# A two-layer network behind channel attention: the first layer from seven block products instead of eight

## What is computed

```python
# q, k, v: (2, 6016, 256); w_in: (256, 2048); w_out: (2048, 256); alpha: (2048,)
qn = q / (norm of q over the 6016 tokens + 1e-6);  kn the same for k
s = kn.transpose(0, 2, 1) @ qn / tau          # 256 x 256 for each batch
a = softmax(s, last axis)
x = (v @ a).reshape(12032, 256)
h = x @ w_in
g = np.maximum(h, 0) + alpha * np.minimum(h, 0)
y = g @ w_out                                  # (12032, 256)
```

## Time and profile before

| | |
|---|---|
| median of three runs | 1151.94 us (1149.97 to 1152.36) |
| span of the profiled execution, first to last instruction | 1147.4 us |
| PE busy | 1134.5 us, 99% of the span |
| DVE busy | 840.3 us, 73% |
| ACT busy | 551.0 us, 48% |
| DMA | 54.6 MB, 13.0% of 16 engines |

### The profile page before, as it was taken

The page is one execution under the profiler, slowest core; times in us unless marked ns, Lnnn a source line. Parts: engine busy times, 40 slices in busy tenths (PEclk is TensorE's granted clock), DMA queues, the critical chain, the costliest instruction groups (busy, mean ns, idle before and its releaser), DMA issues.

```text
span 1147.4 us, 15404 instructions
## 1 busy us (share of the span) xinstructions
PE 1134.5 (99%) x5218; PEld 952.6 (83%) x5220; DVE 840.3 (73%) x1297; ACT 551.0 (48%) x944; POOL 1.3 (0%) x8
## 2 busy tenths in 40 slices
PE   8999999999999999999999999999999999999998
PEld 6778888888888888888898888888888888888888
DVE  5788768678687696876867777767667667667666
ACT  5664545536455454454544544444444444444443
POOL 0000000000000000000000000000000000000000
PEclk9999999999999999999999999999999999999999
DMA  8720210202102012012011010110110110110100
GB/s 307 297 92 1 74 67 9 73 0 73 73 0 73 27 46 73 0 73 73 0 37 33 1 37 1 37 37 0 37 37 0 37 37 0 37 37 0 37 19 15
DMA packets 15308, 54.63 MB, mean 48 GB/s; under 512 B 1584, under 2 KB 2096, under 8 KB 12336
## 3 DMA queue, kind: packets, MB, share of 16 engines
q1 hardware_dynamic: 15280, 54.28, 13.0%
HBM read 41.95 MB, written 12.32 MB: 47 GB/s over the span
## 4 chain that ended last, share of the span: by engine, by line
PE 93%; DVE 3%; DMA 2%; ACT 1%; issue 1%; SPq 0%; ACTq 0%; DVEq 0%
PE y_ps L444 43%; PE h_ps L423 43%; PE s_ps L345 3%; DMA stage<-qk 2%; PE s_ps L323 2%; PE h_ps L392 1%; DVE g L761 1%; DVE g_lo L647 1%; PE small_ps L392 0%; DVE g_hi L771 0%; DVE acc L683 0%; ACT sq L547 0%; DVE sq L713 0%; ACT h_pos L584 0%; DVE col L717 0%
## 5 line engine op out<-in xcount | busy, mean ns | idle before, releaser
L761 DVE SCALAR_TENSOR_TENSOR g<-h_neg,neg_alpha,h_pos 128x512 f32<-128x512 f32 (+1 forms) x384 | 284.1, 740 | 222.6 <-ACT h_neg L585 205.5
L584 ACT ACTIVATE h_pos<-h_ps 128x512 f32<-128x512 f32 (+1 forms) x384 | 226.6, 590 | 453.8 <-PE h_ps L423 282.5
L444 PE MATMUL y_ps<-g_hi,w_hi 128*128 128x512 f32 (+1 forms) x768 | 296.5, 386 | 1.3 <-DVE g_lo L647 1.3
L444 PE MATMUL y_ps<-g_hi,w_lo 128*128 128x512 f32 (+1 forms) x768 | 295.8, 385 | 0.0
L444 PE MATMUL y_ps<-g_lo,w_hi 128*128 128x512 f32 (+1 forms) x768 | 295.3, 384 | 0.0
L647 DVE TENSOR_TENSOR g_lo<-g,g_hi 128x512 fp32r<-128x512 f32 (+1 forms) x384 | 261.8, 682 | 13.3
L585 ACT ACTIVATE h_neg<-h_ps 128x512 f32<-128x512 f32 (+1 forms) x384 | 224.6, 585 | 0.0
L771 DVE CAST g_hi<-g 128x512 fp32r<-128x512 f32 (+1 forms) x384 | 161.9, 422 | 34.6
L444 PEld LDWEIGHTS y_ps<-g_hi,w_hi 128*128 128x128 f32 x768 | 144.3, 188 | 28.4 <-DVE g_lo L647 2.2
L444 PEld LDWEIGHTS y_ps<-g_lo,w_hi 128*128 128x128 f32 x768 | 144.2, 188 | 27.7
L444 PEld LDWEIGHTS y_ps<-g_hi,w_lo 128*128 128x128 f32 x768 | 144.4, 188 | 25.8
(11 more groups left out here) (85 smaller groups left out, 647.9 us busy)
## 6 DMA issues: line engine op xcount, KB each, us to landing
stage<-qk SPq DMA_DIRECT2D x23, 1024.0 KB, 6.3
v_stage<-v_tiles SPq DMA_DIRECT2D x24, 512.0 KB, 3.8
y_t<-y_stage SPq DMA_DIRECT2D x22, 512.0 KB, 3.0
y_stage<-w_pieces SPq DMA_DIRECT2D x8, 512.0 KB, 5.8
stage<-qk SPq DMA_DIRECT2D x2, 512.0 KB, 4.5
y_t<-y_stage SPq DMA_DIRECT2D x2, 384.0 KB, 2.5
tau_sb<-tau_col SPq DMA_DIRECT2D x1, 0.5 KB, 5.0
alpha_sb<-alpha_cols SPq DMA_DIRECT2D x1, 8.0 KB, 5.2
```

Source lines behind the costliest of these rows:

```text
L444: product = nc.tensor.matmul(y_ps[oc][:, 0:width], w_part[:, piece, ws], g_part[:, j % GBUF, 0:width], start=(j == 0 and w_part is w_hi an ...
L584: nc.scalar.activation(h_pos[:, 0:width], h, ACT.Relu)
L761: nc.vector.scalar_tensor_tensor(out=g[:, 0:width], in0=h_neg[:, 0:width], scalar=neg_alpha[:, j:j + 1], in1=h_pos[:, 0:width], op0=ALU.mu ...
```

## The change

The kernel is rewritten around a different unit of work. A tile is now two halves of 512 tokens (1024 tokens; 6 tiles for each batch, the last one with halves of 448). A **group** is one tile and one pair of feature blocks (`jp`, 8 per tile, 96 groups in all). The up product of a group is a 2 x 2 by 2 x 2 block product: features × channels by channels × tokens. It is done by Strassen's method (Winograd's form) with 7 block products of three matmuls each, and no longer with 8:

- `mix_m` forms four sums of M's blocks (S1 to S4) and `mix_v` four sums of v's blocks (T1 to T4) on DVE. ACT and DVE split all seven operands on each side.
- Four products are added up, one after the other, in one PSUM bank X. ACT copies the running sum out after each (`take_x`, L572), since each is a part of one of the four results. Bank Y gets one product, bank Z two, one on top of the other; DVE adds them to what ACT took (`add_part`, L767).
- The slope becomes max(h, alpha·h) on DVE (`slope`, L775), one instruction from SBUF. Where alpha is above 1, signs are turned by a factor `sigma`, which is also put on w_out.
- The layer's second product (`down`, L406) runs one group behind, in four parts that stand between the seven up products.
- M is made by exact fp32 matmuls, 8 steps of 4 (`make_m`, L378); for batch 2 one step stands in each of the groups 41 to 48. The q·k products of batch 2 are exact too: 11 blocks in the head (`late_blocks`), 18 pairs of blocks at the end of groups 8 to 25. The norms and the softmax of batch 2 stand in groups 32 to 37.
- All loops are unrolled. The loads come in other pieces: q and k of batch 1 in 13, v as two per tile, w_in whole (2 MB) before the first `make_m`, w_out in four parts.

The diff of what the prediction speaks of:

```diff
-                    for j in range(FJ):
-                        up(j)
...
-                        if j >= LAG:
-                            down(j - LAG)
+            for G in range(GROUPS):
+                T, jp = G // JP, G % JP
+                if jp == 0:
+                    pe.wait_ge(v_lo_ready, NOP * (T + 1))
+                if T % TILES == 0:
+                    pe.wait_ge(m_lo_ready, JP * (T // TILES) + jp + 1)
+                if G > 0:
+                    pe.wait_ge(c11_done, G)
...
+                up(T, jp, Y, A12, B21, True).then_inc(y_done, 1)
...
+                    pe.wait_ge(x_copied, 4 * G)
+                up(T, jp, X, A11, B11, True).then_inc(x_done, 1)
+                if G > 0:
+                    pe.wait_ge(c12_done, G)
+                up(T, jp, Z, S1, T1, True).then_inc(z_done, 1)
+                if G > 0:
+                    down(G - 1, 0)
+                pe.wait_ge(x_copied, 4 * G + 1)
+                up(T, jp, X, S2, T2, False).then_inc(x_done, 1)
+                if G in M_AT:
+                    pe.wait_ge(c11_done, G + 1)
+                    pe.wait_ge(slice_loaded[M_AT[G] % 2], 16 * (M_AT[G] // 2 + 1))
+                    make_m(Y, w_slice[:, M_AT[G] % 2, :, :])
...
+                if G > 0:
+                    down(G - 1, 1)
+                pe.wait_ge(x_copied, 4 * G + 2)
+                up(T, jp, X, S3, T3, False).then_inc(x_done, 1)
+                if G > 0:
+                    down(G - 1, 2)
+                pe.wait_ge(x_copied, 4 * G + 3)
+                up(T, jp, X, A22, T4, False).then_inc(x_done, 1)
+                pe.wait_ge(c22_done, G + 1)
+                up(T, jp, Z, S4, B22, False).then_inc(z_done, 1)
+                if G > 0:
+                    down(G - 1, 3)
```

```diff
+            def take_x(G, n, k):                       # ACT
...
+                act.wait_ge(x_done, 4 * G + n + 1)
+                if G > 0:
+                    act.wait_ge(g_lo_ready, 4 * (G - 1) + k + 1)
...
+                nc.scalar.mul(h[:, k, 0:H], X[:, 0:H], sigma[:, j:j + 1]).then_inc(x_copied, 1)
...
+                take_x(G, 0, 0)
+                if G > 0:
+                    split_g_hi(G - 1, 3)
+                if jp == 1 and T > 0:
+                    take_y(T - 1, 1)
+                take_x(G, 1, 3)
...
+                if G in M_AT:
+                    take_m(1, M_AT[G])
+                take_x(G, 2, 1)
+                split_g_hi(G, 0)
+                take_x(G, 3, 2)
+                split_g_hi(G, 1)
+                split_g_hi(G, 2)
+                if jp == 0 and T > 0:
+                    take_y(T - 1, 0)
+                if G in M_AT:
+                    split_m_hi(1, M_AT[G])
+                if G in W_OUT_AT:
+                    split_w_hi(W_OUT_AT[G])
```

```diff
+        W_OUT_AT = {2 * n - 1: n for n in range(1, FJ // 4)}
+        V_DVE = {1: (B11, "T1"), 2: (B22, "T3"), 3: (T1, "T2"), 4: (T3,), 5: (T2, B21, "T4"), 7: (T4,)}
...
+            mix_m(0, 0)                                # DVE, batch 1
+            for jp in range(JP):
+                if jp + 1 < JP:
+                    mix_m(0, jp + 1)
+                split_m_lo(0, jp)
+            dve.wait_ge(sigma_ready, 1)
+            split_w_lo(0)
```

More of the change, by code:

```diff
@@ L164, in blocks @@
[L164 to L176, removed]
-        def tiles(eng, b, body):
-            body(0, 0, 0, True, False)
-            with eng.Fori(0, PAIRS) as i:
-                body(i * 2 + 1, i, 1, False, False)
-                body(i * 2 + 2, i + 1, 0, False, False)
-            body(TILES - 1, TILES // 2 - 1, 1, False, True)
@@ L186, in groups @@
[L186 to L196 removed]
+        v_mixed = sem("v_mixed")
+        v_hi_ready = sem("v_hi_ready")
+        v_lo_ready = sem("v_lo_ready")
+        x_done = sem("x_done")
+        y_done = sem("y_done")
@@ L297, in _ @@
+            store(ALL - 1, 0)
+            store(ALL - 1, 1)
+            for t in range(2):
+                sp.wait_ge(y_stored[t], 16 * ALL)
         @block.gpsimd
@@ L351, in channel_sums, with late_blocks @@
-            def channel_sums(b):
-                pe.wait_ge(folded, b + 1)
+                        s_ps[b][:, kc * C:(kc + 1) * C], rows[:, C + kc * P:C + (kc + 1) * P], rows[:, 0:C],
+                        start=False, stop=last, skip_group_check=True)
+                return product
+            def late_blocks(n0, n1):
+                for n in range(n0, n1):
+                    for part in range(len(LATE_PARTS)):
+                        if n == sum(LATE_PARTS[:part]):
+                            pe.wait_ge(late_loaded[part], 16)
+                    product = qk_block(1, late[:, n, :], False)
+                    if n == LATE - 1:
+                        product.then_inc(qk1_summed, 1)
@@ L354, in channel_sums @@
+            def channel_sums(b):
+                acc = (acc0, acc1)[b]
+                if b == 0:
+                    pe.wait_ge(acc0_done, len(SUBS))
+                else:
+                    pe.wait_ge(acc1_done, len(LATE_SUBS) + PAIRS)
                 for n in range(2 * CC):
-                    sums = nc.tensor.matmul(sums_ps[:, n:n + 1],
-                                            acc[:, n // CC, 0, (n % CC) * P:(n % CC + 1) * P],
-                                            ones[:, 0:1], start=True, stop=True)
+                    for half in range(2):
+                        sums = nc.tensor.matmul(sums_ps[:, n:n + 1], acc[:, half, n * P:(n + 1) * P],
+                                                ones[:, 0:1], start=half == 0, stop=half == 1)
@@ L490, in _, with make_m @@
-            product.then_inc(qk_summed, 1)
-            for b in range(B):
-                make_m(b)
-                tiles(pe, b, body(b))
+                moved.then_inc(at_moved, 1)
+            def make_m(bank, w_of):
+                for kc in range(CC):
+                    for qc in range(CC):
+                        product = nc.tensor.matmul(
+                            bank[:, kc * 2 * P:(kc + 1) * 2 * P], at[:, qc, kc * P:(kc + 1) * P], w_of[:, qc, :],
+                            start=qc == 0, stop=qc == CC - 1, skip_group_check=True)
+                product.then_inc(m_done, 1)
@@ L496, in _ @@
+            for k in range(4):
+                down(GROUPS - 1, k)
         @block.scalar
         def _(act):
-            def square(n, t, b, slot, nblk, anew):
-                if not anew:
-                    act.wait_ge(acc_done, t * 2 + (2 * TILES * b + n - 1))
-                nc.scalar.activation(sq[:, n, 0:nblk, :], stage[:, slot, n, 0:nblk, :],
-                                     ACT.Square).then_inc(sq_ready, 1)
-            def split_v(T, par):
-                act.wait_ge(v_loaded, T * 16 + 16)
-                nc.scalar.copy(v_hi[:, par, :, :], v_stage[:, :, :]).then_inc(v_hi_ready, 1)
@@ L636, in _ @@
+            split_g_hi(GROUPS - 1, 3)
+            for t in range(2):
+                take_y(ALL - 1, t)
         @block.vector
```

999 lines of the change are left out of this document (524 added, 475 removed).

## The result

The change takes **1210.22 us** (median of 4 runs, 1207.3 to 1213.03), against 1152.03 us before, measured beside it: ratio 1.051, 95% interval 1.049 to 1.0531. It is slower, as forecast, but 22 us above the forecast's 1188 and 8 us above the likeliest case's own range (1172 to 1202). It lies in the range of 1160 to 1212 by 2 us, and two of the four runs (1212.7 and 1213.03) do not. By its number it is nearest to the rival of the missing spare (1205, 0.12), which the trace excludes, and 8 us from the rival *the clock falls at every pause* (1218, 0.05), to which the trace points.

A forecast was written before the change was run, and what follows sets the result against it. PE's count of matmuls was taken as the bound. 88.3 us to X2, 1008.0 of remaining PE work and waits (13.7, 29.6, 33, 3.5, 1.2, 1.4, 4.4) gave a 1183.1 span; 4.5 more made 1188, range 1160 to 1212.

The forecast's parts named there:

- the likeliest case: Whole kernel: the forecast as walked, 1188 us with 1172 to 1202 as its own range, chance 0.66.
- the rival of the missing spare: Plain groups: the 0.3 us spare before Z2 is absent, some 85 groups stall 0.2 each, +17, 1205 us; chance 0.12.
- the clock falls at every pause: PE's pauses of 2.9 us and more, some 19 places: half speed costs 1.6 each, +30, 1218 us; chance 0.05.
- A plain group: A group without extra work: runs in 10.20 us without a stall, tightest spare 0.3 us before Z2.
- DVE drains faster: DVE's slopes, additions and splits: follow each other at 0.43 us, not 0.60 to 0.66; 38 less, 1150 us; chance 0.14.
- Tile starts: Eleven tile starts: Y waits for v's last split, 2.9 us each, 3.3 behind a q·k pair, sum 29.6.
- Batch 2's M: Groups 41 to 49: the chain of sums, cast and split delays the fourth `g_lo` and `make_m`, sum 33 us.
- Batch 1's M: Head: two buffers, 3.2 us a part; X2 starts at 88.3, PE idles 12.1 us.
- Tile 0: First tile: uncovered copies, slow clock, squares, additions and w_out pieces delay its groups, sum 13.7 us.
- I add 8 x 0.2 = 1.6: Tile 0, after the pause behind batch 1's M: first matmuls at the 1.2 GHz level cost 1.6 us.
- The 4.5 us from span to median: Whole kernel: the runs' median stands 4.5 us above the span, taking 1183.1 to 1188.
- It does not save matmuls: Whole kernel: rival that matmuls are not saved; excluded, since PE's order has 45 in a group.

The follow-up runs named there:

- experiment 6: The changed kernel with zero matmuls in the pause behind batch 1's M, at each tile start and in groups 41 to 48: 1194.13 us.
- experiment 5: The changed kernel with zero matmuls in PE's waits in the groups around batch 2's M, 8 ahead of X2 and 5 ahead of `make_m`: 1203.52 us.
- experiment 3: The changed kernel with 45 zero matmuls in the pause behind batch 1's M: 1204.7 us.
- experiment 2: The changed kernel with ten zero matmuls ahead of PE's wait at each tile start: 1204.69 us.
- The fastest version: The changed kernel with splits, squares and sums moved into waits, more buffers for both batches' M, and 20 zero matmuls behind batch 1's M: 1116.15 us.
- experiment 4: The changed kernel with two buffers for batch 2's M, its sums and splits one group after `make_m`: 1175.38 us.

## Why the prediction was right and where not

The sum can be held against the trace stretch by stretch, from one start of a Y product in the timeline to another (us; the first column is put together from the terms of the sum and, rounded, adds up to 1183.9; the last is experiment 6):

| stretch | walked | the change | experiment 6 |
|---|---|---|---|
| start to tile 1 | 179.0 | 181.7 | 182.3 |
| tile 1 | 100.2 | 100.9 | 99.4 |
| tile 2 | 100.2 | 101.1 | 99.4 |
| tile 3 | 88.5 | 91.0 | 88.2 |
| tile 4 | 89.4 | 91.6 | 90.1 |
| groups 40 to 49 | 140.5 | 156.1 | 145.9 |
| groups 50 to 55 | 64.1 | 64.2 | 64.2 |
| tiles 7 to 10 | 340.0 | 341.2 | 341.1 |
| tile 11 to the end | 82.0 | 83.7 | 84.1 |

- **A plain group, 10.20.** Measured 10.20. The rival *the spare is not there* falls: in plain groups neither X3 nor Z2 waits. Pair groups 11.94 (11.97 walked).
- **Slope and additions.** They have the duration of the instruction taken for them. By line and form, x count | busy us, mean ns:

```profile
L775 DVE SCALAR_TENSOR_TENSOR h<-h,alpha_sb 128x512 f32<-128x512 f32 x320 | 232.2, 747 | 2.8
L767 DVE SCALAR_TENSOR_TENSOR h<-z_ps,sigma,h 128x512 f32<-128x512 f32 x160 | 120.1, 751 | 146.8 <-ACT h L572 145.9 <-PE z_ps L386 0.9
L767 DVE SCALAR_TENSOR_TENSOR h<-p_ps,sigma,h 128x512 f32<-128x512 f32 x80 | 59.6, 746 | 0.0
L760 DVE TENSOR_TENSOR m_lo<-mf,m_hi 128x896 fp32r<-128x896 f32 x16 | 17.4, 1089 | 8.0 <-ACT m_hi L560 8.0
```

  So the rival *DVE drains faster* falls. Reading PSUM costs no more than SBUF here: 751 and 746 against 747 ns. The surcharge that the Trainium skill gives (VectorE: DVE Perf Modes, TRN2 errata) isn't seen in this instruction. The 896-wide split was walked at 1.09 and takes 1.089.
- **Tile starts, 2.9 each.** 2.7 to 2.8 (12.97 - 10.20) eight times, 3.36 (15.3 - 11.94) for the two behind a q·k pair, 3.3 walked, all released by `v_lo` as said. The eleventh is group 48's.
- **Batch 2's M.** The walk gives 93.8 us for the groups 42 to 47 with the wait at group 48's start (6 x 10.79 of matmuls + 23.1 + 6.0). At full clock they take 94.6, in experiments 5 and 6 both. The fourth `g_lo` of group 42 ends 6.98 us into the next group (620.23 of 613.25, experiment 5's group 43), walked 5.8 + 2 x 0.54 = 6.88. ACT's copy ahead of X2, for which the walk had nothing, costs next to nothing at full clock, since `make_m` right behind it waits longer. So the stall was sized rightly; in the change, with the clock's fall, the same groups take 105.7.
- **Batch 1's M.** X2 at 89.09 for 88.3, parts 3.12 us apart for 3.2.
- **Tile 0.** Walked stalls 3.4, 3.2, 1.0 and 2.3 in groups 1, 2, 4 and 6; measured 3.4, 3.9, 1.0 and 2.4.
- **What failed** is the step "I add 8 x 0.2 = 1.6", and with it the 0.05 for the clock at every pause. I put the clock's fall into the sum once, where it was known that PE had stood still for 12 us, and took a wait of 1.81 us with full speed behind it as evidence for all the others. The tile starts' were longer, 2.54 us and up, and at the starts of tiles 1 to 5 half speed stood behind them; in groups 42 to 47 it stood behind waits of 1.4 to 2.4 us and a second one for `make_m`. Set stretch by stretch against experiment 6, the change loses to it 2.7 us in the head behind M (3.3 against experiment 3), 7.3 in tiles 1 to 4 and 10.2 in groups 40 to 49, and 14.4 there if group 48 is put at experiment 2's 11.79. So the clock cost 20 to 24 of the 28 us in this execution, where the sum had 1.6; by the medians, with group 48's zero matmuls in the way, it is 16. In a sum with twelve pauses, each longer than the 1.81 us on which it relied, that rival should have had a third or more of the chances.
- The rest, 4 to 8 us, lies in small excesses, tile 11's 1.7 the largest, which no run took apart.
- **The 4.5 us from span to median** was too much: in the runs of the change and of the experiments the time stands 1.7 to 1.9 us above the span (2.7 in one). It hides 2.7 us of the miss.
- **What was luck.** The range reached 1212 to take in the missing spare, which isn't there, and by that the clock's 20 us and more fell just inside it. The direction, the tile starts, the head's pause and batch 2's M were right by their mechanism; that 1210 lies within the range was not earned.
- *It does not save matmuls*: excluded, and so it was. The fastest version takes 1116 us with 13 us of waits left in PE's list, so "without waits about 1095" was some 8 us too low.

## What to carry to other kernels

When a change cuts the bottleneck engine's work by a few per cent, walk the other engines' queues at each edge (a tile's start, a phase that shares its buffers): the last instruction before the edge, and the buffer with one copy, decide more than the count of matmuls. Work that is wanted early goes into a wait of its queue that is there in any case, not to a group's end. And price each new wait of TensorE twice, once for its length and once for half speed behind it. A wait as long that shows full speed after it does not rule this out: here equal waits had either behind them.

## What the runs showed that I had not expected

- A wait of the same 2.61 us was followed by the 1.2 GHz level at the start of tile 1 and by 2.4 GHz at the start of tile 7. Even one place goes both ways. Tile 7 in the change is shown above; in experiment 4, whose code at that place is the same, PE's timeline has:

```profile
750.83 0.69 PE L388 MATMUL p_ps<-v_hi,m_hi 128*128 128x512 f32 x1 [2.61 <-DVE v_lo L680]
751.31 0.63 PE L388 MATMUL p_ps<-v_lo,m_hi 128*128 128x512 f32 x1
751.74 0.63 PE L388 MATMUL p_ps<-v_hi,m_lo 128*128 128x512 f32 x1
```

- The same code goes both ways from one execution to the next. Experiment 5 edits nothing ahead of group 41, and its waits at the starts of tiles 1 to 4 are the change's (2.61, 3.01, 3.01 and 2.61 us). Yet the clock stayed full behind all four, and their first groups take 11.91, 11.87, 11.87 and 12.38 us for 13.32, 13.51, 14.65 and 13.79:

```profile
182.58 0.50 PE L386 MATMUL p_ps<-v_hi,m_hi 128*128 128x512 f32 x1 [2.61 <-DVE v_lo L685]
...
180.00:560.00 380.00, 364.41 (x1606) 298.89 (x1606) 287.72 (x434) 205.10 (x329) 0.00 (x0) 1.00 0.14 46
```

  That is 7 us, as much as one filling's whole effect, and the four runs of the change differ by 6 us, the two slower ones with a mean clock of 0.968, the others with 0.976 and 0.973. So what the single fillings (experiments 2, 3 and 5) gained is known only within some us, and that tiles 1 and 2 kept the clock in experiment 3 need not come from the filled head. The length of one wait doesn't settle it; what does was not found.
- Zero matmuls need not cover a wait: in experiment 2 they left 8.5 of the 32.4 us at tile starts open, and the clock stayed up behind all eleven. That is not certain either: at group 48's start 3.40 us were left there, and in experiment 6, with 3.43 us left, the first matmuls ran at half speed.
